# Adding an attention mask with VectorE while it reduces the row, instead of with TensorE into PSUM

## The chip, the cores and the metric

The kernel runs on one core of one Trainium2 chip. The metric is the device time of one execution in microseconds (us); for the kernel before it is the median of 3 runs.

## The reference

Three stages follow each other. The first is sliding window attention with sinks, and only this one is touched by the change: 2 batches, 8 heads, 768 positions, head size 64, everything in float32. A query sees the keys less than 128 positions behind it, and the first 4 keys.

```python
scores = scale * np.matmul(q, k.transpose(0, 1, 3, 2))
keep = is_sink | in_window
scores = np.where(keep, scores, -1000000000.0)
scores = scores - np.max(scores, axis=-1, keepdims=True)
a = np.exp(scores)
a = a / (np.sum(a, axis=-1, keepdims=True) + 1e-09)
return np.matmul(a, v).astype(np.float32)
```

The second stage turns the attention's output by the angle `x @ w_theta`, mixes tokens with two 768 x 768 matrices and adds a ReLU branch. The third is a gated block with a 512 x 1024 input matrix, a layer norm, a 768 x 768 mixing over tokens and an output matrix.

## The kernel before

Every engine has a program of its own, and semaphores order them. The attention goes over 8 blocks: four pairs of heads, and for each pair the two batches (function `pair(n, b, last, with_tok)` in the programs of TensorE, VectorE and ScalarE). A block has 6 tiles of 128 queries. Both heads of a pair lie side by side, head h on partitions 64h to 64h+63 of the transposed q and k. Tile i is scored against 128 keys (i = 0), 256 keys (i = 1) or 288 (i of 2 and more: two blocks of 128 keys, and 32 columns for the sinks).

For one tile the work passes through the engines so:

1. TensorE, `scores` (L1139): into the PSUM buffer `s_ps[i % 2]`, for each head first a matmul of the bf16 identity `ident_b` with the bf16 mask `BIAS[i]` (0 or -1e9; L1148), then three matmuls for q and k, each split in a high and a low float32r part (L1154).
2. VectorE, `maxima` (L836): per head one `tensor_reduce` with max and negation (L839) gives `neg_max`.
3. ScalarE, `exps` (L560): per head `exp(score + neg_max)` with the row's sum in its accumulator (L564).
4. TensorE, `turn_probs`: transposes of the probabilities (L1164, L1166). ScalarE copies head 0 (L581) and VectorE head 1 (L858) to SBUF, and TensorE multiplies by v (`times_v`, L1176 for the sinks, L1181).
5. VectorE, `weights` and `normalise`: the divisor (L862, L864), the product (L871).

The programs are written out by hand in an order that has the scores of tile i+2 made while tile i is transposed. In the first six blocks (`with_tok`) each of the steps i = 0 to 3 also turns a piece of the token matrices: TensorE transposes it (L1204), ScalarE writes its high part (`tok_high`, L576), VectorE its low part (`tok_low`, L853). VectorE's order in such a step is `copy_pt`, `tok_low` of the step before, `weights`, `maxima`, `normalise`; ScalarE's is `copy_pt`, `exps`, `tok_high`. TensorE's transposes of piece j wait for the low part of piece j-1.

At a block's end, q and k of the next are transposed (L1136), and ScalarE (`q_high` L551, `k_high` L558) and VectorE (`q_low` L827, `k_low` L834) split them. Scores of its tiles 0 and 1 are made between the transposes of x. These go to `x_t` by L610 (ScalarE) and L913 (VectorE), and TensorE's last transposes of k wait for both.

The first two blocks are written out on all three engines. Blocks 2 to 5 are a loop in hardware of two turns (`Fori(1, PAIRS - 1)`), in which semaphore values and addresses come from registers. Blocks 6 and 7 are written out.

GpSimd makes the identity and `ident_b` (L446), loads w_theta, and splits it with one copy (L453) and one subtraction (L455) near the start. VectorE makes the mask (L816 to L820), ahead of its first `q_low`. TensorE waits for `ident_b` before its first transpose (L1257) and for the mask ahead of its first scores (L1267).

Of the kernel before, what the change touches and what calls it, by code (L numbers as in the profile page):

```python
# [6 lines left out]
F32 = mybir.dt.float32  # L7
F32R = mybir.dt.float32r
BF16 = mybir.dt.bfloat16
I32 = mybir.dt.int32  # L10
ACT = mybir.ActivationFunctionType
ALU = mybir.AluOpType
AX = mybir.AxisListType

BATCH, HEADS, SEQ, HD = 2, 8, 768, 64
P = 128
# [8 lines left out]
PAIRS = HEADS // 2  # L25
HALFSEQ = SEQ // 2
# [3 lines left out]
SINKS = 32  # L30
WIN = 2 * P
STEP = P + SINKS
K_COLS = 2 * P + (TILES - 2) * STEP
SCALE = 1.0 / math.sqrt(HD)
NEG = 1.0e9
DEN_EPS = 1e-9
VAR_EPS = 1e-6

# [6 lines left out]
def attn_moe_gmlp(nc, q, k, v, n_sink, window, w_theta, w_tok_r, w_tok_i, w_ch, w_in, w_spatial, b_spatial,  # L45
                  w_out, out):
    ctx = ExitStack()
    with ctx:
        def sem(name):
            return ctx.enter_context(nc.semaphore(name))  # L50

        def at(name, offset, shape, dt):
            return nc.alloc_sbuf_tensor_at(name, shape, dt, offset=offset)
# [11 lines left out]
        const_at = stage_at + 2 * SEQ * 4  # L65
# [41 lines left out]
        rel = at("rel", o, [P, WIN], F32)  # L107
        col = at("col", o + 1024, [P, WIN], F32)
        keep_w = at("keep_w", o + 2048, [P, WIN], F32)
        keep_s = at("keep_s", o + 3072, [P, WIN], F32)  # L110
        keep_1 = at("keep_1", o + 4096, [P, WIN], F32)
        o += 5120
        bias_0 = at("bias_0", o, [P, P], BF16)
        bias_1 = at("bias_1", o + 256, [P, WIN], BF16)
        bias_2 = at("bias_2", o + 768, [P, SINKS + WIN], BF16)
# [8 lines left out]
        q_hi, q_lo = (at(f"q_{w}", o + 3072 * j, [P, SEQ], F32R) for j, w in enumerate(("hi", "lo")))  # L124
# [48 lines left out]
        stage = [at(f"stage{b}", stage_at + SEQ * 4 * b, [P, SEQ], F32) for b in range(2)]  # L173
        b_row = at("b_row", stage_at, [P, SEQ], F32)
        ident = at("ident", const_at, [P, P], F32)
        ident_b = at("ident_b", const_at + 512, [P, P], BF16)
        small = const_at + 768
        lims_i = at("lims_i", small, [P, 4], I32)
        words = at("words", small + 32, [P, 4], F32)
# [3 lines left out]
        neg_max = at("neg_max", small + 64, [P, 2, 2], F32)  # L183
# [11 lines left out]
        s_ps = banks[0:2]  # L195
# [4 lines left out]


        s_ident = sem("ident_made")
        s_identb = sem("ident_b_made")
        s_lims = sem("limits_loaded")
        s_iota = sem("iota_made")
        s_mask = sem("mask_steps")
        s_bias = sem("bias_made")
# [7 lines left out]
        s_qhi = sem("q_hi_ready")  # L215
# [4 lines left out]
        s_max = sem("max_ready")  # L220
# [95 lines left out]
        def ncols(i):  # L316

            return P if i == 0 else WIN + (SINKS if i >= 2 else 0)
# [21 lines left out]
        BIAS = [bias_0, bias_1] + [bias_2] * (TILES - 2)  # L340
# [91 lines left out]
        def _(pool):  # L432
            pool.memset(ident[:, :], 0.0).then_inc(s_ident, 1)
            for b in range(2):
# [7 lines left out]
                      allow_small_or_imprecise_dtypes=True).then_inc(s_iota, 1)  # L442
            pool.iota(col[:, :], pattern=[[1, WIN]], base=0, channel_multiplier=0,
                      allow_small_or_imprecise_dtypes=True).then_inc(s_iota, 1)
            pool.wait_ge(s_ident, 2)
            pool.tensor_copy(ident_b[:, :], ident[:, :]).then_inc(s_identb, 1)  # L446


            pool.wait_ge(s_k, 32)
# [95 lines left out]
        def _(act):  # L545
            def q_high(g, t, unit, src=tr_ps):

                act.wait_ge(s_tr, t + 1)
                if unit is not None:
                    act.wait_ge(s_sc, 2 * unit)  # L550
                act.activation(q_hi[:, g * HALFSEQ:(g + 1) * HALFSEQ], src[:, 0:HALFSEQ], ACT.Copy,  # L551
                               scale=SCALE).then_inc(s_qhi, 1)

            def k_high(g, t, bank=tr_ps):

# [4 lines left out]
            def exps(m, i, b):  # L560

                for h in range(2):
                    act.wait_ge(s_max, 2 * m + h + 1)
                    act.activation(probs[i % 2][:, 0:ncols(i), h], s_ps[i % 2][:, h, 0:ncols(i)], ACT.Exp,  # L564
                                   bias=neg_max[:, i % 2, h:h + 1],
                                   accum_out=sums[:, (TILES * b + i) % 4, h:h + 1]).then_inc(s_exp, 1)

            def x_high(n, j):
# [218 lines left out]
        def _(dve):  # L787
# [25 lines left out]
            dve.tensor_tensor(keep_1[:, :], keep_w[:, :], keep_s[:, :], ALU.max).then_inc(s_mask, 1)  # L813
            dve.tensor_tensor(rel[:, 0:P], keep_w[:, P:WIN], keep_s[:, 0:P], ALU.max).then_inc(s_mask, 1)
            dve.wait_ge(s_mask, 5)
            dve.tensor_scalar(bias_0[:, :], rel[:, 0:P], -1.0, NEG, ALU.add, ALU.mult).then_inc(s_bias, 1)  # L816
            dve.tensor_scalar(bias_1[:, :], keep_1[:, :], -1.0, NEG, ALU.add, ALU.mult).then_inc(s_bias, 1)
            for c, dst in ((0, 0), (P, STEP)):
                dve.tensor_scalar(bias_2[:, dst:dst + P], keep_w[:, c:c + P], -1.0, NEG, ALU.add, ALU.mult).then_inc(s_bias, 1)
            dve.tensor_scalar(bias_2[:, P:STEP], keep_s[:, 0:SINKS], -1.0, NEG, ALU.add,  # L820
                              ALU.mult).then_inc(s_bias, 1)

            def q_low(g, no, src=tr_ps):

                dve.wait_ge(s_qhi, 2 * no + g + 1)
                cols = slice(g * HALFSEQ, (g + 1) * HALFSEQ)
                dve.scalar_tensor_tensor(q_lo[:, cols], src[:, 0:HALFSEQ], SCALE, q_hi[:, cols].bitcast(F32), ALU.mult,  # L827
                                         ALU.subtract).then_inc(s_qlo, 1)

            def k_low(g, no, bank=tr_ps):  # L830
# [4 lines left out]

            def maxima(m, i):  # L836
                for h in range(2):
                    dve.wait_ge(s_sc, 2 * m + h + 1)
                    dve.tensor_reduce(neg_max[:, i % 2, h:h + 1], s_ps[i % 2][:, h, 0:ncols(i)], AX.X, ALU.max,  # L839
                                      negate=True).then_inc(s_max, 1)  # L840

            def x_low(n, j):

# [80 lines left out]
                maxima(i, i)  # L924
            for b in range(2):
                pair(0, b, False, True)
            with dve.Fori(1, PAIRS - 1) as n:
                for b in range(2):
                    pair(n, b, False, True)
            pair(PAIRS - 1, 0, False, False)  # L930
# [3 lines left out]
            with dve.If(dve.value_load(general[0:1, 0:1]) > 0):  # L934
# [11 lines left out]
                with dve.Fori(0, PAIRS) as n:  # L946
                    for b in range(2):
                        m = (2 * n + b) * TILES
                        for i in range(TILES):
# [13 lines left out]
                            for h in range(2):  # L963
# [9 lines left out]
                                                  negate=True).then_inc(s_g_max, 1)  # L973
# [54 lines left out]
            for j in range(4):  # L1028
                b, turn = j % 2, GT // 2 - 2 + j // 2
                dve.wait_ge(s_z[b], 2 * turn + 1)  # L1030
                tile = slice(GT - 4 + j, GT - 4 + j + 1)
# [94 lines left out]
        def _(pe):  # L1126
# [12 lines left out]
            def scores(m, i, pair_no):  # L1139

                pe.wait_ge(s_qlo, 2 * pair_no + i // 3 + 1)
                pe.wait_ge(s_klo, 4 * pair_no + (1, 1, 3, 4, 4, 4)[i])
                if not (isinstance(m, int) and m < 2):
                    pe.wait_ge(s_exp, 2 * m - 2)
                keys = slice(k_col(max(i - 1, 0)), k_col(max(i - 1, 0)) + ncols(i))
                tile = slice(i * P, (i + 1) * P)
                for h in range(2):
                    pe.matmul(s_ps[i % 2][:, h, 0:ncols(i)], ident_b[:, :], BIAS[i][:, :], start=True, stop=False)  # L1148

                for q_part, k_part in ((q_lo, k_hi), (q_hi, k_lo), (q_hi, k_hi)):  # L1150
                    for h in range(2):
                        rows = slice(h * HD, (h + 1) * HD)
                        last = q_part is q_hi and k_part is k_hi
                        mm = pe.matmul(s_ps[i % 2][:, h, 0:ncols(i)], q_part[rows, tile], k_part[rows, keys], start=False,  # L1154
                                       stop=last)
                        if last:
                            mm.then_inc(s_sc, 1)
# [96 lines left out]
                    turn(k_raw, 3)  # L1254

            pe.wait_ge(s_ident, 2)
            pe.wait_ge(s_identb, 1)  # L1257

            pe.wait_ge(s_q, 32)
            turn(q_raw, 0)  # L1260
# [3 lines left out]
            turn(q_raw, 3, pt_ps[:, 1, :])  # L1264
            pe.wait_ge(s_qlo, 1)
            turn(k_raw, 3)
            pe.wait_ge(s_bias, 5)  # L1267
            for i in range(2):
                scores(i, i, 0)
            pe.wait_ge(s_qlo, 2)  # L1270
# [10 lines left out]
            with pe.If(pe.value_load(general[0:1, 0:1]) > 0):  # L1281
                with pe.Fori(0, PAIRS) as n:
                    for b in range(2):
                        m = (2 * n + b) * TILES
                        pe.wait_ge(s_g_load, 96 * (2 * n + b) + 96)
                        for g in range(4):
# [4 lines left out]
                            for j in range(3):  # L1291
                                mm = pe.transpose(tr_ps[:, j * P:(j + 1) * P], (g_q_raw, g_k_raw)[g // 2][:, g % 2 * 3 + j, :],
                                                  ident[:, :])
                            mm.then_inc(s_g_tr, 1)
                        pe.wait_ge(s_g_trc, 4 * (2 * n + b) + 4)
                        for i in range(TILES):
                            for h in range(2):
                                u = 2 * (m + i) + h
                                rows = slice(h * HD, (h + 1) * HD)
# [147 lines left out]
```

## Time and profile before

| | before |
| --- | --- |
| device time, median of 3 runs (lowest to highest) | 525.67 us (524.82 to 526.9) |
| the profiled execution: span from first to last instruction | 532.6 us |
| mean granted TensorE clock in that span | 0.958 |
| busy: TensorE matmuls / weight loads | 497.1 us (93%) / 431.1 us (81%) |
| busy: VectorE / ScalarE / GpSimd | 254.8 us (48%) / 188.7 us (35%) / 123.9 us (23%) |
| chain that ended last: TensorE / VectorE / ScalarE | 76% / 11% / 5% |

The profile is one execution, another than the three timed ones. Its time outside the span isn't given, so its own time is known only as no less than 532.6 us, 5.7 us above the slowest of the timed runs. The attention takes about 197 us of the span. Busy matmuls overlap each other in the records. The chain of waits is followed back from the last instruction, and shows which work set the end in each stretch. The granted clock is the share of 2.4 GHz that TensorE was granted: 1.00 is 2.4 GHz, 0.50 is 1.2 GHz.

### The profile page before, as it was taken

To read this page: it belongs to the slowest core of one execution; us is meant where nothing else is said; L and a number is where in the kernel's file an instruction comes from. 1 tells how busy PE (TensorE), PEld (TensorE's weight loads), DVE (VectorE), ACT (ScalarE), POOL (GpSimd) and SP (SyncE) were. 2 spreads that over 40 slices of the span, in tenths; PEclk is the share of its full clock that TensorE was granted. 3 is DMA by queue.
4 is the path that set the end of the run, shared out by engine and by line. 5 is a ranking of instruction groups with operands and counts; after the bars stand their busy time and mean duration, and the time that the engine had idled before them with its cause. 6 is when DMAs were issued, how large, how long until landed. Compare 5 with 4: busy or idle time off the path is not lost.

```text
span 532.6 us, 8197 instructions
## 1 busy us (share of the span) xinstructions
PE 497.1 (93%) x2844; PEld 431.1 (81%) x2844; DVE 254.8 (48%) x591; ACT 188.7 (35%) x474; POOL 123.9 (23%) x93
## 2 busy tenths in 40 slices
PE   3899999989989997879999999999999999999997
PEld 2687877868768775659999999988888888999885
DVE  5744676767766738996000010475262540333222
ACT  2523565554644715663111111254142321110220
POOL 2500000000000002686544443000000007443442
PEclk9955999999999997897999999999999999999999
DMA  8603251651422000000420000120010110000122
GB/s 212 136 30 77 74 121 40 142 100 49 90 50 43 0 5 2 0 0 1 144 94 1 0 0 0 33 87 1 0 60 0 32 76 1 0 0 0 41 98 98
DMA packets 44527, 25.83 MB, mean 48 GB/s; under 512 B 39248, under 2 KB 39248, under 8 KB 44496
## 3 DMA queue, kind: packets, MB, share of 16 engines
q1 hardware_dynamic: 43152, 20.19, 15.1%
q0 software_dynamic: 1344, 5.24, 2.8%
q8 instruction: 17, 0.28, 0.2%
q14 instruction: 14, 0.11, 0.1%
HBM read 22.28 MB, written 3.15 MB: 48 GB/s over the span
## 4 chain that ended last, share of the span: by engine, by line
PE 76%; DVE 11%; ACT 5%; issue 5%; POOL 1%; DMA 1%; SPq 0%; DVEq 0%; ACTq 0%; POOLq 0%
PE ps L1129 18%; PE ps L1130 18%; PE ps L1131 18%; PE ps L1181 6%; PE ps L1136 4%; PE ps L1154 4%; PE ps L1164 3%; ACT probs L564 2%; PE ps L1176 2%; DVE red L1007 2%; PE ps L1148 2%; DVE neg_max L839 1%; ACT tok_hi L576 1%; DVE tok_lo L853 1%; DVE xtl L845 1%
## 5 line engine op out<-in xcount | busy, mean ns | idle before, releaser
L1129 PE MATMUL ps<-tok_hi,zl 128*128 128x384 f32 x192 | 65.4, 341 | 4.5 <-POOL zl L485 4.5
L1130 PE MATMUL ps<-tok_lo,zh 128*128 128x384 f32 x192 | 65.3, 340 | 0.0
L1131 PE MATMUL ps<-tok_hi,zh 128*128 128x384 f32 x192 | 65.2, 340 | 0.0
L564 ACT ACTIVATE probs<-ps,neg_max 128x288 f32<-128x288 f32 (+2 forms) x96 | 45.6, 488 | 38.8 <-DVE neg_max L839 38.3
L1181 PE MATMUL ps<-v_raw,p_t 128*128 128x64 f32 x352 | 52.9, 295 | 1.4 <-issue 1.4
L1181 PEld LDWEIGHTS ps<-v_raw,p_t 128*128 128x128 f32 x352 | 46.1, 203 | 8.3 <-issue 4.9
L1039 DVE TENSOR_TENSOR x_t<-ps,x_t 128x768 f32 (+1 forms) x8 | 7.7, 958 | 80.1 <-PE ps L1131 80.1
L466 POOL COPY x_sb<-xs 128x768 f32 x8 | 6.6, 827 | 163.5 <-DVE xs L871 163.5
L1129 PEld LDWEIGHTS ps<-tok_hi,zl 128*128 128x128 f32 x192 | 37.0, 193 | 4.9 <-issue 4.9
L839 DVE TENSOR_REDUCE neg_max<-ps 128x1 f32<-128x288 f32 (+2 forms) x96 | 36.0, 416 | 4.7 <-PE ps L1154 4.4
L1130 PEld LDWEIGHTS ps<-tok_lo,zh 128*128 128x128 f32 x192 | 36.9, 192 | 0.0
L1131 PEld LDWEIGHTS ps<-tok_hi,zh 128*128 128x128 f32 x192 | 36.9, 192 | 0.0
L1164 PE MATMUL ps<-ident,probs 128*128 128x128 f32 x176 | 32.4, 305 | 1.5 <-ACT p_t L581 1.3
L1129 PE MATMUL ps<-sp_hi,vl 128*128 128x384 f32 x96 | 32.2, 335 | 0.7 <-ACT gate_t L749 0.7
L1130 PE MATMUL ps<-sp_lo,vh 128*128 128x384 f32 x96 | 32.1, 334 | 0.0
L1131 PE MATMUL ps<-sp_hi,vh 128*128 128x384 f32 x96 | 32.1, 334 | 0.0
L1164 PEld LDWEIGHTS ps<-ident,probs 128*128 128x128 f32 x176 | 26.6, 209 | 3.0 <-ACT probs L564 2.2
L520 POOL TENSOR_TENSOR vl<-vn_sb,vh 128x768 fp32r<-128x768 f32 x8 | 19.5, 2444 | 38.2 <-ACT vh L717 38.2
L1107 DVE TENSOR_TENSOR mixed<-ps,b_row 128x768 f32<-128x768 f32 x8 | 7.7, 957 | 43.1 <-PE ps L1131 43.1
L858 DVE COPY p_t<-ps 128x384 f32<-128x384 f32 (+2 forms) x48 | 23.4, 488 | 9.1 <-PE ps L1166 4.8
L1129 PE MATMUL ps<-th_hi,xtl 128*128 128x512 f32 x48 | 21.2, 442 | 6.6 <-DVE red L1013 6.0
L475 POOL TENSOR_TENSOR zi_sb<-x_sb,sin_x 128x512 f32 (+1 forms) x12 | 16.4, 1368 | 29.1 <-ACT cos_x L668 29.1
(146 smaller groups left out, 1131.3 us busy)
## 6 DMA issues: line engine op xcount, KB each, us to landing
q_raw<-in_q SPq DMA_DIRECT2D x16, 192.0 KB, 3.1
k_raw<-in_k SPq DMA_DIRECT2D x16, 192.0 KB, 3.7
v_raw<-in_v SPq DMA_DIRECT2D x16, 192.0 KB, 3.2
out<-o_sb SPq DMA_DIRECT2D x12, 256.0 KB, 2.0
stage<-in_moe_w_tok_r SPq DMA_DIRECT2D x6, 384.0 KB, 3.4
stage<-in_moe_w_tok_i SPq DMA_DIRECT2D x6, 384.0 KB, 3.0
stage<-in_moe_w_spatial SPq DMA_DIRECT2D x6, 384.0 KB, 3.4
in_raw<-in_moe_w_in POOLq DMA_DIRECT2D x1, 2048.0 KB, 9.5
```

Of the source, the lines that this page charges most:

```text
L475: pool.tensor_tensor(zi_sb[:, tile, :], x_sb[:, tile, :], sin_x[b][:, :].rearrange("p (o n) -> p o n", o=1), ALU.mult).then_inc(s_z[b], 1)
L520: pool.tensor_tensor(vl[b][:, :, :], vn_sb[:, b * TILES:(b + 1) * TILES, bass.ds(n * P, P)], vh[b][:, :, :].bitcast(F32), ALU.subtract).th ...
L564: act.activation(probs[i % 2][:, 0:ncols(i), h], s_ps[i % 2][:, h, 0:ncols(i)], ACT.Exp, bias=neg_max[:, i % 2, h:h + 1], accum_out=sums[: ...
L839: dve.tensor_reduce(neg_max[:, i % 2, h:h + 1], s_ps[i % 2][:, h, 0:ncols(i)], AX.X, ALU.max, negate=True).then_inc(s_max, 1)
L858: dve.tensor_copy(p_t[i % 2][1][:, 0:pt_cols(i, 1)], pt_ps[:, 1, 0:pt_cols(i, 1)]).then_inc(s_ptc[1], 1)
L1129: pe.matmul(dst, w_lo, m_hi, start=first, stop=False)
L1130: pe.matmul(dst, w_hi, m_lo, start=False, stop=False)
L1131: return pe.matmul(dst, w_hi, m_hi, start=False, stop=last)
L1136: mm = pe.transpose(dst[:, j * P:(j + 1) * P], src[:, base + j, :], ident[:, :])
L1154: mm = pe.matmul(s_ps[i % 2][:, h, 0:ncols(i)], q_part[rows, tile], k_part[rows, keys], start=False, stop=last)
L1164: mm = pe.transpose(pt_ps[:, h, dst:dst + P], probs[i % 2][:, c:c + P, h], ident[:, :])
L1181: mm = pe.matmul(o_ps[:, cols], p_t[i % 2][h][:, c:c + P], v_raw[b][:, t, cols], start=(i < 2 and j == 0), stop=(j == len(blocks(i)) - 1 a ...
```

## The change

The mask is no longer put into PSUM by TensorE. The scores are made negated, since q is scaled by `-SCALE`, and the mask holds 0 or +1e9. VectorE adds the mask to the scores in place in PSUM and takes the row's minimum in the same instruction, which is `neg_max`. ScalarE computes `exp(-score + neg_max)`. `tensor_tensor_reduce(out, in0, in1, scale, scalar, op0, op1, accum_out)` computes `out = (in0 op0 in1) * scale` and `accum_out = reduce(out, op1)` from the starting value `scalar`.

```diff
+LARGE = 3.0e38
-            pool.wait_ge(s_ident, 2)
-            pool.tensor_copy(ident_b[:, :], ident[:, :]).then_inc(s_identb, 1)
...
                 act.activation(q_hi[:, g * HALFSEQ:(g + 1) * HALFSEQ], src[:, 0:HALFSEQ], ACT.Copy,
-                               scale=SCALE).then_inc(s_qhi, 1)
+                               scale=-SCALE).then_inc(s_qhi, 1)
...
-                                   bias=neg_max[:, i % 2, h:h + 1],
+                                   scale=-1.0, bias=neg_max[:, i % 2, h:h + 1],
...
             def maxima(m, i):
                 for h in range(2):
+                    dve.wait_ge(s_bias, 5)
                     dve.wait_ge(s_sc, 2 * m + h + 1)
-                    dve.tensor_reduce(neg_max[:, i % 2, h:h + 1], s_ps[i % 2][:, h, 0:ncols(i)], AX.X, ALU.max,
-                                      negate=True).then_inc(s_max, 1)
+                    dve.tensor_tensor_reduce(s_ps[i % 2][:, h, 0:ncols(i)], s_ps[i % 2][:, h, 0:ncols(i)], BIAS[i][:, :], 1.0,
+                                             LARGE, ALU.add, ALU.min, neg_max[:, i % 2, h:h + 1]).then_inc(s_max, 1)
...
-            with dve.Fori(1, PAIRS - 1) as n:
+            for n in range(1, PAIRS - 1):
                 for b in range(2):
                     pair(n, b, False, True)
...
-                for h in range(2):
-                    pe.matmul(s_ps[i % 2][:, h, 0:ncols(i)], ident_b[:, :], BIAS[i][:, :], start=True, stop=False)
-
                 for q_part, k_part in ((q_lo, k_hi), (q_hi, k_lo), (q_hi, k_hi)):
...
-                        mm = pe.matmul(s_ps[i % 2][:, h, 0:ncols(i)], q_part[rows, tile], k_part[rows, keys], start=False,
+                        mm = pe.matmul(s_ps[i % 2][:, h, 0:ncols(i)], q_part[rows, tile], k_part[rows, keys], start=q_part is q_lo,
                                        stop=last)
...
-            pe.wait_ge(s_identb, 1)
...
-            pe.wait_ge(s_bias, 5)
```

The scale of `q_low` and the mask's factor in L816 to L820 change sign too. VectorE's program for blocks 2 to 5 is written out; TensorE and ScalarE keep their loop.

## Rows read from the trace of the kernel before

**Rows 1.** The chain of waits up to 245 us, shares of that stretch by line.

```profile
by line: PE ps L1181 13.1%; issue 9.9%; PE ps L1136 8.7%; PE ps L1154 8.0%; PE ps L1164 6.2%; ACT probs L564 4.6%; PE ps L1176 4.2%; DVE red L1007 3.4%; PE ps L1148 3.3%; DVE neg_max L839 3.2%; ACT tok_hi L576 2.7%; DVE tok_lo L853 2.5%; DV
```

**Rows 2.** Instructions by line and shape: count, busy us, mean ns, idle before.

```profile
L839 DVE TENSOR_REDUCE neg_max<-ps 128x1 f32<-128x288 f32 x64 | 26.2, 450 | 2.9 <-PE ps L1154 2.6
...
L853 DVE TENSOR_TENSOR tok_lo<-ps,tok_hi 128x384 f32 x16 | 8.9, 558 | 8.3 <-ACT tok_hi L576 8.3
...
L1010 DVE TENSOR_TENSOR ps<-ps,red 128x512 f32<-128x512 f32 x12 | 7.7, 684 | 0.0
```

**Rows 3.** Timeline near the start: start us, us, engine, line.

```profile
16.88 4.54 POOL L455 TENSOR_TENSOR th_lo<-th_raw,th_hi 128x2048 fp32r<-128x2048 f32 x1
18.89 2.57 DVE L862 TENSOR_SCALAR den<-sums 128x2 f32<-128x2 f32 x1
```

**Rows 4.** Stretches: us, TensorE busy (count), granted clock, DMA share, GB/s.

```profile
24.00:25.00 1.00, 0.76 (x6) 0.95 0.00 0
...
52.00:53.00 1.00, 1.00 (x11) 0.89 1.34 220
```

**Rows 5.** Chain of waits, 24 to 52 us: start us, us, what.

```profile
25.64 0.48 PE ps L1148 x2
...
29.45 0.64 PE ps L1204 x3
...
46.12 0.50 ACT x_t L610
...
51.17 0.48 PE ps L1148 x2
```

**Rows 6.** Timeline of one step in block 3, in the loop.

```profile
98.41 0.82 DVE L839 TENSOR_REDUCE neg_max<-ps 128x1 f32<-128x288 f32 x2
98.90 0.52 ACT L564 ACTIVATE probs<-ps,neg_max 128x288 f32<-128x288 f32 x1 [1.16 <-DVE neg_max L839]
99.31 0.19 ACT L564 ACTIVATION_READ_ACCUMULATOR probs<-ps,neg_max 128x1 f32 x1
99.40 0.51 ACT L564 ACTIVATE probs<-ps,neg_max 128x288 f32<-128x288 f32 x1
99.88 0.49 ACT L576 ACTIVATE tok_hi<-ps 128x384 f32 x1
100.53 0.56 DVE L853 TENSOR_TENSOR tok_lo<-ps,tok_hi 128x384 f32 x1 [0.56 <-ACT tok_hi L576]
101.31 0.82 DVE L839 TENSOR_REDUCE neg_max<-ps 128x1 f32<-128x288 f32 x2
```

**Rows 7.** Timeline of part of a step in block 1, which is written out.

```profile
56.74 0.49 ACT L576 ACTIVATE tok_hi<-ps 128x384 fp32r<-128x384 f32 x1
57.32 0.55 DVE L853 TENSOR_TENSOR tok_lo<-ps,tok_hi 128x384 fp32r<-128x384 f32 x1
58.06 0.80 DVE L839 TENSOR_REDUCE neg_max<-ps 128x1 f32<-128x288 f32 x2
```

**Rows 8.** Chain of waits from block 1 to 6.

```profile
58.90 0.33 PE ps L1204 x3
...
68.54 0.50 ACT x_t L610
...
97.78 0.04 DVEq L863
...
109.24 0.11 PE ps L1148 x2
...
110.31 0.22 PE ps L1148 x2
...
113.45 0.42 PE ps L1148 x2
...
160.54 0.25 PE ps L1148 x2
```

**Rows 9.** Timeline: ScalarE's copy to x_t at the end of block 3.

```profile
111.67 0.49 ACT L610 ACTIVATE x_t<-ps 128x384 f32 x1 [0.28 <-PE ps L1136]
```

More of the change, by code:

```diff
@@ L175, in attn_moe_gmlp @@
         ident = at("ident", const_at, [P, P], F32)
-        ident_b = at("ident_b", const_at + 512, [P, P], BF16)
         small = const_at + 768
@@ L202, in attn_moe_gmlp @@
         s_ident = sem("ident_made")
-        s_identb = sem("ident_b_made")
         s_lims = sem("limits_loaded")
@@ L815, in _ @@
             dve.wait_ge(s_mask, 5)
-            dve.tensor_scalar(bias_0[:, :], rel[:, 0:P], -1.0, NEG, ALU.add, ALU.mult).then_inc(s_bias, 1)
-            dve.tensor_scalar(bias_1[:, :], keep_1[:, :], -1.0, NEG, ALU.add, ALU.mult).then_inc(s_bias, 1)
+            dve.tensor_scalar(bias_0[:, :], rel[:, 0:P], -1.0, -NEG, ALU.add, ALU.mult).then_inc(s_bias, 1)
+            dve.tensor_scalar(bias_1[:, :], keep_1[:, :], -1.0, -NEG, ALU.add, ALU.mult).then_inc(s_bias, 1)
             for c, dst in ((0, 0), (P, STEP)):
-                dve.tensor_scalar(bias_2[:, dst:dst + P], keep_w[:, c:c + P], -1.0, NEG, ALU.add, ALU.mult).then_inc(s_bias, 1)
-            dve.tensor_scalar(bias_2[:, P:STEP], keep_s[:, 0:SINKS], -1.0, NEG, ALU.add,
+                dve.tensor_scalar(bias_2[:, dst:dst + P], keep_w[:, c:c + P], -1.0, -NEG, ALU.add, ALU.mult).then_inc(s_bias, 1)
+            dve.tensor_scalar(bias_2[:, P:STEP], keep_s[:, 0:SINKS], -1.0, -NEG, ALU.add,
                               ALU.mult).then_inc(s_bias, 1)
@@ L826, in q_low @@
                 cols = slice(g * HALFSEQ, (g + 1) * HALFSEQ)
-                dve.scalar_tensor_tensor(q_lo[:, cols], src[:, 0:HALFSEQ], SCALE, q_hi[:, cols].bitcast(F32), ALU.mult,
+                dve.scalar_tensor_tensor(q_lo[:, cols], src[:, 0:HALFSEQ], -SCALE, q_hi[:, cols].bitcast(F32), ALU.mult,
                                          ALU.subtract).then_inc(s_qlo, 1)
```

## The prediction

> **What bounds the kernel now.** The page's busy shares put TensorE at 93%, but they average over stages, so I read the chain of waits for the attention alone. There the mask's matmuls (L1148) hold 3.3% of 245 us, 8.1 us, and VectorE's maxima (L839) 3.2% [rows 1]. The change takes away the first and makes the second longer, so the question is on which stretches each is on the path. The chain by stretches gives four kinds.
>
> Before 21.5 us GpSimd decides. Its subtraction for w_theta takes 4.54 us, and VectorE's small `den` instruction behind it takes 2.57 us instead of 0.16: it ends when GpSimd does [rows 3].
>
> From 24.9 to 52.1 us the granted clock is 0.50, that is 1.2 GHz [rows 4], and the chain runs through TensorE almost alone.
>
> From 70 to 157 us, in blocks 2 to 5, the steps with token pieces are a ring between VectorE and ScalarE: max of head 0, exp of head 0 (0.49 us later), exp of head 1 (0.50), `tok_hi` (0.48), `tok_lo` (0.65), the divisor and the next max (0.78). It takes 2.90 us, from 98.41 to 101.31 [rows 6]. The chain goes that way 16 times, without one L1148. Only at the blocks' ends does it go through TensorE, with 0.11 and 0.22 us of L1148 [rows 8].
>
> In block 1, and in blocks 6 and 7 without token pieces, TensorE binds, with 0.24 or 0.25 us of L1148 per tile [rows 8].
>
> **What the removal gives.** I go by the pieces of L1148 on the chain. On the ring they are worth nothing.
> - Before 21.5 us: three pieces, 1.23 us together. Worth 0, for `den` still waits for GpSimd, whose subtraction waits for a DMA and not for TensorE. The copy to `ident_b` and the two moved waits are worth 0 too: the mask stands ahead of `q_low` in VectorE's program, so TensorE's scores come after it in any case. The repeated wait for `s_bias` is always met.
> - At 1.2 GHz: five pieces, from 25.64 to 51.17 us, 2.08 us [rows 5]. There TensorE's step is over 4 us against the ring's 2.90, so all of it counts: -2.1.
> - Six transitions (into blocks 2 to 7), 0.33 us each [rows 8]. Next in line is ScalarE's `x_t` copy, which has 0.28 us of idle ahead of it [rows 9], and its `exp` comes behind the longer max (below: 0.14 us). Left are 0.28 - 0.14 = 0.14 us each: -0.8 (bounds 0 and -2.0).
> - The first scores of two blocks, about 0.4 us each [rows 8]. VectorE's `p_t` copy is next, and the max itself grows: 0.2 each, -0.4.
> - Block 1 at 2.4 GHz: two pieces, 0.49 us, against three longer maxima once the ring takes over: 0.
> - Blocks 6 and 7: six pieces like the one at 160.54 [rows 8]: -1.5. VectorE has some 2.0 us of work there in a step of 2.5, so the longer instructions fit.
>
> **What the new instruction costs.** No row shows it. It reads PSUM and the mask, writes PSUM and hands out an extreme. Two-source instructions that read PSUM take 558 ns for 384 columns and, in place, 684 ns for 512: 0.98 ns per column, so 464 ns at 288, against 450 for the reduction [rows 2]. That is 0.01 us more. The second wait costs VectorE's queue one slot, 0.04 us, as L863's does [rows 8]. Handing out the extreme costs nothing if it comes with the instruction. ScalarE's counterpart is an instruction of its own of 0.19 us, and the next starts 0.09 us after it [rows 6]. So the max becomes later by x, between 0 (reading and writing more can't be quicker) and 0.01 + 0.04 + 0.19 = 0.24 us. I take the spacing of the one counterpart there is: x = 0.01 + 0.04 + 0.09 = 0.14.
>
> The Trainium skill ("VectorE: DVE Perf Modes", section "Two Vector instructions with no wait between them") says that a Vector instruction which also writes out its accumulator is two instructions, the main one and an accumulator read. By it the lower end would drop out and the sum below would lie at 0.14 or above; if it didn't hold here, x would be 0.05. No VectorE row shows it.
>
> **What the written-out program gives.** In the loop `tok_lo` starts 0.65 us after `tok_hi`, in written-out block 1 0.58; from `tok_lo` to the max it is 0.78 against 0.74 [rows 6, 7]. So registers cost the ring 0.07 + 0.04 = 0.11 us per step, and VectorE's part of that goes in blocks 2 to 5. Sixteen passes: 16 x (0.14 - 0.11) = +0.5. This part hides most of the new instruction's price.
>
> **The sum.** -2.1 - 0.8 - 0.4 - 1.5 + 0.5 = -4.3 us. The span of 532.6 us is 6.9 above the runs' median of 525.67; I take the difference over to the median: 521.4. Ends of x: at 0 the terms are -2.1 - 2.0 - 0.8 - 0.5 - 1.5 - 1.8 = -8.7, so 517.0; at 0.24 they are -2.1 - 0.2 + 0.3 - 1.5 + 2.1 = -1.4, so 524.3. The stages behind the attention only move.
>
> **Rivals.**
>
> *The low clock lasts longer* (slower). TensorE falls to 1.2 GHz at 24.9 us, after a stretch with holes (busy 0.76 of the last microsecond), and comes back at 52.1 [rows 4], in the midst of two tiles of scores. The change takes the full-height matmuls out of just that stretch, and leaves a wider hole ahead of 21.5 us. Nothing in the rows says that it comes back at the same place. From the last token piece to `x_t` a block takes 46.12 - 29.45 = 16.67 us at 1.2 GHz and 68.54 - 58.90 = 9.64 at 2.4 [rows 5, 8]: 7.0 more, 6.7 without the masks. Its four steps add from 1 to 2 us each where TensorE takes over from the ring, or less in the lighter first ones: 10 us for one more block, 531.4. It decides once the low stretch is longer by about half a block. Against it: after 52.1 the clock stays at 1.00 through the attention.
>
> *The clock comes back earlier or isn't lost.* By the same rows block 0's end would give 6.7 and its last step some 1 more: 514.
>
> *The instruction is dearer than its parts.* Each 0.1 us on x falls on 16 ring passes, 3 of block 1 and 6 transitions: 2.5 us. The gain is gone at x = 0.31, where the 288 columns take 0.76 us with the wait. At x = 0.4 it is 527.9. For it: no such instruction is in the trace. Against: twice as long as any two-source row says.
>
> *The removed matmuls were cover only.* If the chain's 0.25 us pieces are the array's changeover to half-height weights, which stays, and the transitions are held by ScalarE, no gain is left outside the low stretch, and that one is absorbed with the clock: 525.7.
>
> **Chances.** Forecast 0.48 (517.0 to 524.3), longer low clock 0.20 (531.4), dearer instruction 0.10 (524 to 530), cover only 0.12 (525.7), better clock 0.10 (514). A measurement of this kernel tells 0.5%, 2.6 us, from no change. Below 523.0 lie 0.40 of the forecast and the better clock: faster 0.50. Within: 0.08, the cover 0.12 and 0.02 of the dear instruction: 0.22. Slower: 0.20 + 0.08 = 0.28. The range from 514 to 531 leaves out about half of the longer low clock and some of the better one.
>
> **What the new profile would show.** Right: no L1148; TensorE idle ahead of token pieces in blocks 2 to 5; ring steps of 2.9 us; blocks 6 and 7 shorter by some 0.25 us a step; from max to exp about 0.63 us; the clock's return near 50 us. Wrong: a low clock past 60 us or none at all, an instruction over 0.7 us, or steps of blocks 6 and 7 unchanged.

## The result, and the profile after

The changed kernel takes 530.87 us (median of 8 executions, 528.1 to 549.9); the kernel of before, run beside it, 525.68 us (8 executions, 524.2 to 534.7). The ratio is 1.0086 [1.006, 1.0111]: slower by 0.9%, where 521.4 us had been forecast. It is outside "no change" and just inside the upper end of the range, 531.

One thing about the executions has to be known to read what follows: those of one and the same kernel differ by how long TensorE runs at 1.2 GHz, and the ratios leave out every execution more than 1.5% above its kernel's fastest.

The profiled execution of the changed kernel took 549.85 us, its span 548.0. These are the head of its page and the lines that answer to the kernel of before's:

```profile
span 548.0 us, 8067 instructions
...
PE 511.0 (93%) x2748; PEld 442.3 (81%) x2748; DVE 260.0 (47%) x687; ACT 188.6 (34%) x474; POOL 124.5 (23%) x92
...
PEclk9856999999965558797999999999999999999999
```

The row of clocks has two deep dents: slices 2 to 4 (14 to 55 us) and slices 12 to 15 (about 151 to 206 us). The kernel of before had only the first; shallower ones (digits 7 and 8) lie behind the attention in both. In stretches of the trace (us, TensorE busy and its instructions, granted clock, DMA share, GB/s) the edges are these:

```profile
24.00:25.00 1.00, 0.51 (x4) 0.70 0.00 0
27.00:28.00 1.00, 1.00 (x8) 0.50 0.00 0
...
51.00:52.00 1.00, 1.00 (x10) 0.65 1.32 233
52.00:53.00 1.00, 1.00 (x11) 1.00 1.34 218
...
154.00:155.00 1.00, 0.78 (x4) 0.55 1.17 264
155.00:156.00 1.00, 1.00 (x8) 0.50 1.20 249
207.00:208.00 1.00, 1.00 (x3) 0.50 0.00 0
208.00:209.00 1.00, 1.00 (x4) 0.64 0.00 0
209.00:210.00 1.00, 1.00 (x6) 1.00 0.00 0
```

The first fall and the return lie half a microsecond ahead of where [rows 4] has them: 24.4 and 51.7 us. The second low stretch, from 154.1 to 208.7 us, is new. Ahead of it TensorE was busy for 0.33 of the microsecond from 151 and 0.36 of that from 153:

```profile
151.00:152.00 1.00, 0.33 (x4) 1.00 0.00 0
152.00:153.00 1.00, 1.00 (x9) 1.00 0.00 0
153.00:154.00 1.00, 0.36 (x6) 1.00 0.31 72
```

Such holes alone don't bring it: in a quick execution of the same kernel (below) TensorE is busy for 0.45, 0.88, 0.55 and 0.58 of the microseconds from 142, at the same place of the program, and the clock stays at 1.00.

What that costs stands on the chain of waits, where ScalarE's copy to `x_t` ends each block (start us, us, what):

```profile
46.02 0.50 ACT x_t L607
...
151.38 0.50 ACT x_t L607
...
181.15 0.50 ACT x_t L607
...
213.77 0.49 ACT x_t L607
```

Block 0 ends as before (46.12, [rows 5]), though three of the removed pieces, 1.12 us, lie ahead of that. They are used up by a token transpose that starts at 24.71 us and not at 24.24 (GpSimd's subtraction is 0.37 us later here), and by the fall at 24.4 and not at 24.9: the transposes from there take 1.72 us for 1.18. At 151.38 the changed kernel is 3.5 us ahead: the kernel of before has this copy at 154.93. Then blocks 6 and 7 take 29.8 and 32.6 us, where they took 19.5 and 22.6. That is +20.25 us; behind the attention 1.3 us are gained (334.2 us against 335.5). So -3.55 + 20.25 - 1.3 = +15.4, the difference of the spans (548.0 - 532.6).

The new instruction, by line and shape, and one step of block 3 in the timeline:

```profile
L837 DVE CUSTOM_DVE_ANT_0 ps<-ps,bias 128x288 f32<-128x288 f32 x64 | 28.2, 482 | 4.2 <-PE ps L1149 3.8 <-issue 0.3
L837 DVE DVE_READ_ACCUMULATOR2_ANT neg_max<- 128x1 f32 x96 | 13.6, 141 | 0.0
```

```profile
111.72 0.47 DVE L837 CUSTOM_DVE_ANT_0 ps<-ps,bias 128x288 f32<-128x288 f32 x1
...
112.10 0.14 DVE L837 DVE_READ_ACCUMULATOR2_ANT neg_max<- 128x1 f32 x1
112.10 0.50 DVE L837 CUSTOM_DVE_ANT_0 ps<-ps,bias 128x288 f32<-128x288 f32 x1
112.28 0.51 ACT L561 ACTIVATE probs<-ps,neg_max 128x288 f32<-128x288 f32 x1 [0.39 <-DVE neg_max L837]
...
113.25 0.49 ACT L573 ACTIVATE tok_hi<-ps 128x384 f32 x1
...
113.77 0.56 DVE L851 TENSOR_TENSOR tok_lo<-ps,tok_hi 128x384 fp32r<-128x384 f32 x1 [0.57 <-ACT tok_hi L573]
...
114.56 0.47 DVE L837 CUSTOM_DVE_ANT_0 ps<-ps,bias 128x288 f32<-128x288 f32 x1
```

The instruction is two: 482 ns, and a read of the accumulator of 141 ns with which the next instruction starts. From max to `exp` it is 0.56 us against 0.49 [rows 6], where 0.63 had been expected; the ring takes 2.84 us (111.72 to 114.56) against 2.90. The Trainium skill ("VectorE: DVE Perf Modes", section "Two Vector instructions with no wait between them") had said of such an instruction that it is two. By that the trace agrees; the price, 141 ns, is the trace's.

### The profile page after: what moved, and what is told of

The parts are those of the page before. It is cut to its first block, busy times and chain, and to the rows that moved or that the text cites. A ratio compares the mean times of both kernels' runs of the same rounds, so it can differ in the third digit from the quotient of the medians.

```text
span 548.0 us, 8067 instructions
## 1 busy us (share of the span) xinstructions
PE 511.0 (93%) x2748; PEld 442.3 (81%) x2748; DVE 260.0 (47%) x687; ACT 188.6 (34%) x474; POOL 124.5 (23%) x92
## 4 chain that ended last, share of the span: by engine, by line
PE 77%; DVE 12%; ACT 5%; issue 4%; POOL 1%; DMA 1%; SPq 0%; ACTq 0%; DVEq 0%; POOLq 0%
PE ps L1127 17%; PE ps L1129 17%; PE ps L1128 17%; PE ps L1176 10%; PE ps L1159 4%; PE ps L1149 3%; PE ps L1134 3%; PE ps L1171 3%; DVE red L1005 2%; ACT probs L561 2%; PE ps L1199 2%; DVE ps L1008 1%; DVE red L1001 1%; DVE red L1011 1%; DVE xtl L843 1%
## 5 line engine op out<-in xcount | busy, mean ns | idle before, releaser
L1176 PE MATMUL ps<-v_raw,p_t 128*128 128x64 f32 x352 | 62.9, 333 | 1.5 <-issue 1.5
L1176 PEld LDWEIGHTS ps<-v_raw,p_t 128*128 128x128 f32 x352 | 55.5, 239 | 9.9 <-issue 7.5
L837 DVE CUSTOM_DVE_ANT_0 ps<-ps,bias 128x288 f32<-128x288 f32 (+2 forms) x96 | 39.0, 447 | 5.3 <-PE ps L1149 4.7
L1159 PE MATMUL ps<-ident,probs 128*128 128x128 f32 x176 | 37.2, 342 | 1.8 <-ACT p_t L578 1.2
L1159 PEld LDWEIGHTS ps<-ident,probs 128*128 128x128 f32 x176 | 30.0, 217 | 3.8 <-ACT probs L561 2.4
L869 DVE TENSOR_TENSOR xs<-ps,rden 128x128 f32<-128x128 f32 x48 | 13.9, 290 | 25.5 <-PE ps L1176 25.3
```

The lines of the kernel that those rows point to most:

```text
L837: dve.tensor_tensor_reduce(s_ps[i % 2][:, h, 0:ncols(i)], s_ps[i % 2][:, h, 0:ncols(i)], BIAS[i][:, :], 1.0, LARGE, ALU.add, ALU.min, neg_ ...
L1159: mm = pe.transpose(pt_ps[:, h, dst:dst + P], probs[i % 2][:, c:c + P, h], ident[:, :])
L1176: mm = pe.matmul(o_ps[:, cols], p_t[i % 2][h][:, c:c + P], v_raw[b][:, t, cols], start=(i < 2 and j == 0), stop=(j == len(blocks(i)) - 1 a ...
```

## The experiments

Three theories stood at first. **A, the clock:** without the mask's matmuls TensorE spends more time at 1.2 GHz; at 2.4 GHz the change gains some 3 us. **B, the instruction:** the longer maximum on VectorE holds the attention, whatever the clock. **C:** VectorE's written-out program costs the time. A fourth, **H, the hole**, came up later: the clock is lost through a gap of TensorE's work near 22 us that GpSimd makes. The experiments were run in three groups, each with the kernel of before beside it: 525.75 us in the median of 28 executions (the first four experiments), 526.24 of 24 (the next four) and 526.19 of 28 (the last four).

### The kernel of before again

No edit.

> The kernel before, once more, for a look at an undisturbed execution: the page of before was taken of an execution of about 534.5 us (span 532.6), 9 us above the median. Theory A (the clock): the profile of a 525 us execution has no stretch at 1.2 GHz from 25 to 52 us, or a much shorter one, and the rest of the attention as before; span 523 to 525. Theory B (the instruction) and theory C (the written-out program) say nothing of it: the low stretch would be there in any execution, and the 9 us would lie elsewhere, spread over stages.

524.76 us in the median (10 executions, 522.84 to 536.52), ratio 0.9984 [0.9961, 1.0008]. The profiled execution took 527.05 us, and its clock is another than in the profile that the prediction read:

```profile
24.00:25.00 1.00, 0.50 (x4) 0.64 0.00 0
27.00:28.00 1.00, 1.00 (x9) 0.66 0.00 0
28.00:29.00 1.00, 1.00 (x10) 1.00 0.00 0
```

It is back at 2.4 GHz at 28 us, not at 52, as A had it. (Block 7 of this trace has another short low stretch, from 181.3 to 184.7 us, that the prediction's profile had not.) There is a difference at the start, too, that the granted clock doesn't show, but the length of the matmuls does. A group of three 128x128 transposes here (upper fence, timeline) and in the changed kernel (lower):

```profile
19.35 0.52 PE L1204 MATMUL ps<-ident,stage 128*128 128x128 f32 x3
```

```profile
19.16 0.85 PE L1199 MATMUL ps<-ident,stage 128*128 128x128 f32 x3
```

The changed kernel still runs at the pace of 1.2 GHz here, and reaches the quick one at about 21 us; in this trace of before it is reached by 18 us. That isn't the mask's matmuls alone: of the traces below that have none of them at the start, two reach it by 17.6 us (pieces, late filler), one at 27 and one after 59. Of the 88 executions of the kernel of before that ran beside the others, 61 took 528 us or less and 27 between 533 and 537, none more; with the ten here it is 68 and 30. The page that I had read was of one of the 27: a span of 532.6 us, with some 1.85 us around it 534.5.

### The changed kernel with the mask's matmuls back

```diff
+                for h in range(2):
+                    pe.matmul(s_ps[i % 2][:, h, 0:ncols(i)], ident_b[:, :], BIAS[i][:, :], start=True, stop=False)
...
-  ... k_part[rows, keys], start=q_part is q_lo,
+  ... k_part[rows, keys], start=False,
```

The copy to `ident_b` and the waits come back too. The mask is added twice here.

> The kernel after, with the mask's matmuls put back on TensorE (the mask is then added twice). TensorE has all of its old work, VectorE the new instruction and the written-out program. Theory A (the change lost by low clock that comes with the removed matmuls): 525 to 528 us, with executions spread as those of before. Theory B (the new instruction costs it): the instruction's cost comes on top of all of TensorE's old work, 531 us or more. Theory C (VectorE's written-out program costs it): 531 or more as well.

526.5 us (12 executions, 523.4 to 537.0), ratio 1.0006 [0.9982, 1.0031]. With the matmuls back the executions lie as those of before do: 8 of 12 up to 527.4, 4 from 533 to 537, none, by their times, with a second long stretch of low clock. The new instruction and the written-out program are in this kernel, so neither of them makes the loss; B would have left it. What is left of the difference is the removal.

### The kernel of before without the mask

```diff
-                for h in range(2):
-                    pe.matmul(s_ps[i % 2][:, h, 0:ncols(i)], ident_b[:, :], BIAS[i][:, :], start=True, stop=False)
...
-  ... k_part[rows, keys], start=False,
+  ... k_part[rows, keys], start=q_part is q_lo,
```

This kernel adds no mask at all; VectorE's reduction stays as it was.

> The kernel before with the mask left out altogether: no mask matmul, the plain reduction over unmasked scores, VectorE's loop as before. Only TensorE's removal is left. Theory A: no faster than before, 526 to 531 us, with executions above 535 us more often than before's and stretches at 1.2 GHz in the attention. Theory B: the gain without the price, 519 to 522 us. Theory C: 519 to 522 us as well.

530.68 us in the median of 6 executions: 519.5, 528.9, 530.6, 530.7, 532.3 and 542.1. There are too few alike for a ratio. As A had it. The removal alone does it: the one quick execution is 3.2 us below the quickest of before beside it, and the other five are 9 us or more above that quick one, where 8 of the 28 of before beside it are long; one is longer than any of before.

### The kernel of before, VectorE's program written out

```diff
-            with dve.Fori(1, PAIRS - 1) as n:
+            for n in range(1, PAIRS - 1):
```

> The kernel before, with VectorE's program for blocks 2 to 5 written out and nothing else changed. Theories A and B: 16 ring passes at up to 0.11 us less, 524 us (523.5 to 525.7). Theory C: 529 us or more, with VectorE waiting for nothing that the profile shows.

531.29 us in the median of 11: five from 520.5 to 525.1 us, six from 531.3 to 534.1. The ratio, 0.9941 [0.9916, 0.9965], rests on the five; their quickest took 520.5 us, the quickest of before beside it 522.7. The six long ones are a larger share than before's 8 of 28, and by the median alone C, 529 us or more, would stand. Against C are the five, and the kernel with the mask's matmuls back, written out too, of whose 12 executions 4 are long. Whether writing out makes the low clock more frequent these counts can't tell. The chain has the copies to `x_t` here (upper fence) and in the kernel of before again (lower):

```profile
59.41 0.50 ACT x_t L610
...
142.94 0.50 ACT x_t L610
```

```profile
59.48 0.50 ACT x_t L610
...
145.69 0.50 ACT x_t L610
```

Blocks 2 to 5 take 83.53 us against 86.21, 2.7 less; 0.11 us on each of 16 passes had been reckoned, 1.8. From `tok_hi` to `tok_lo` it is 0.51 us in this trace (86.79 to 87.30) against 0.65 in the loop [rows 6], and the ring takes 2.72 us. Against the kernel with both the new instruction and the mask's matmuls, whose blocks 2 to 5 take 85.87 us, this one shows the instruction alone: 2.34 us, or 0.146 if spread over 16 passes, where x had been 0.14. The pass itself is 2.84 us there, 0.12 more, of which 0.08 lies between max and `exp` (0.56 against 0.48) and 0.04 ahead of the max; the rest of the 2.34 falls at the blocks' starts and on one longer step.

### The changed kernel again

No edit.

> The kernel after, once more, for a look at an undisturbed execution (the page of after was taken of one of 549.85 us). Theory A (the low clock near the start is the rule once the mask's matmuls are gone): matmuls from 20 to 50 us as long as at 1.2 GHz (transposes of the probabilities near 0.42 us against 0.30), whatever clock the records state there, and full speed from about 55 us on; 528 to 531 us. Rival (the loss lies in steps at full clock): matmuls from 20 to 50 us at full speed and blocks 2 to 5 longer than the 21.1 to 21.9 us of before.

519.6, 519.7, 531.1 and 542.4 us. The profiled execution is a quick one and not of the kind that the expectation describes, with a span of 517.8 us and the granted clock at 1.00 through the attention. Its matmuls take as long as at 1.2 GHz until 27 us (a pair of the scores' matmuls takes 0.44 us at 21.68 us and 0.29 at 27.04), and then the short time. This is what the change is worth when the clock stays: 519.6 against 522.6, the quickest of before beside it, so -3.0 us. With the first 8, the changed kernel's 12 executions are 519.6 and 519.7; six from 528.1 to 531.1; and 538.8, 541.3, 542.4 and 549.9. Ten of twelve lose some 8 us or more, against 27 of 88 before. Four are beyond any of before. The second long stretch was seen in the one of 549.9 only; that the other three have one, too, is taken from their times.

### Filler matmuls in the first two blocks

```diff
+                for h in range(2 * REPS):
+                    pe.matmul(s_ps[i % 2][:, h % 2, 0:ncols(i)], ident_b[:, :], BIAS[i][:, :], start=True, stop=True)
                 for q_part, k_part in ((q_lo, k_hi), (q_hi, k_lo), (q_hi, k_hi)):
```

The scores that follow overwrite what the filler writes. Here it is one pair ahead of each of the first 12 tiles: the removed work, back in two blocks, with its result unused.

> The kernel after, with the mask's matmuls kept in blocks 0 and 1 only and as filler: the scores' first matmul overwrites what they wrote, and VectorE adds the mask as in after. Theory A: the start is back as before, with executions near 520 us (519.5 to 522) and, as with before, some near 531. Rival (the loss lies in the new instruction or in steps at full clock): 528 to 531, as after.

Missed. 534.96 us in the median of 14, ratio 1.0008 [0.998, 1.0036]. It rests on six executions, and these are 524.4 to 527.5 us rather than 520. Three lie near 535, five from 542 to 548. The profiled execution has no low clock at the start, though TensorE's hole is there (busy for 0.09 of the microsecond from 22), and a long one late:

```profile
PEclk9999999999855568977999999999999999999999
```

So the late fall doesn't need the early one, and what the first blocks are given doesn't keep it away.

### A denser filler

REPS is 3 for the first six tiles and 1 for the next two.

> As the last one, but with three times the filler in block 0 and one in the first two tiles of block 1. Theory A: 519.5 to 522 us, and fewer executions in the long form than with the single filler, since TensorE's hole at 18 to 24 us, behind GpSimd's subtraction, gets shorter. Rival: 528 to 532, the filler's own time on top.

520.22 us in the median of 12, ratio 0.9928 [0.9889, 0.9967]. Eight lie between 519.8 and 520.3, the other four at 523.2, 527.4, 530.4 and 530.7; none above. Matmuls whose result nobody reads make this kernel quicker: its median was 530.87 us over the twelve executions above, though two of the four run beside this experiment were at 519.6 too. The run doesn't tell A from H, for the filler also fills the hole: TensorE is busy for 0.97, 1.00, 1.00 and 0.80 of the microseconds from 21. Why three pairs on six tiles also keep the late stretch away, and one pair on twelve does not, no run here says.

### GpSimd's subtraction in four pieces

```diff
-            pool.tensor_tensor(th_lo[:, :, :], th_raw[:, :, :], th_hi[:, :, :].bitcast(F32),
-                               ALU.subtract).then_inc(s_th_w, 1)
+            for c in range(KC):
+                part = (slice(None), slice(c, c + 1), slice(None))
+                low = pool.tensor_tensor(th_lo[part], th_raw[part], th_hi[part].bitcast(F32), ALU.subtract)
+            low.then_inc(s_th_w, 1)
```

The rest is the changed kernel, without filler.

> The kernel after, with GpSimd's one 4.5 us subtraction for w_theta in four pieces, so that VectorE's divisor waits for a piece of about 1.1 us and not for the whole, and TensorE's hole behind it closes. If the hole keeps the clock low (theory H): most executions near 519 to 521 us. Theory A in its narrow form (it is the lacking matmuls from 11 to 18 us): the start stays slow as in after, 525 to 529 us, better by the 2 to 3 us of the hole at most.

520.13 us in the median of 8, ratio 0.9899 [0.9866, 0.9933]: five from 518.5 to 520.9, two near 530, one at 540.6. In the timeline VectorE's `den`, which GpSimd's subtraction holds, is this in the quick execution of the changed kernel (first fence) and here (second):

```profile
18.32 3.19 DVE L860 TENSOR_SCALAR den<-sums 128x2 f32<-128x2 f32 x1
```

```profile
17.21 4.97 POOL L454 TENSOR_TENSOR th_lo<-th_raw,th_hi 128x512 fp32r<-128x512 f32 x4
18.62 1.12 DVE L862 TENSOR_SCALAR den<-sums 128x2 f32<-128x2 f32 x1
```

`den` now waits for one piece (1.28 us each) and not for the whole. Elsewhere it takes 0.16 us. TensorE's gap behind it shrinks, in the changed kernel's execution of 549.85 us (first fence) and here (second):

```profile
21.00:22.00 1.00, 0.68 (x7) 1.00 0.63 138
22.00:23.00 1.00, 0.00 (x0) 1.00 0.64 255
23.00:24.00 1.00, 0.85 (x8) 1.00 0.00 0
24.00:25.00 1.00, 0.51 (x4) 0.70 0.00 0
```

```profile
21.00:22.00 1.00, 0.92 (x8) 1.00 0.77 304
22.00:23.00 1.00, 0.50 (x5) 1.00 0.11 40
23.00:24.00 1.00, 1.00 (x11) 1.00 0.00 0
24.00:25.00 1.00, 0.89 (x9) 1.00 0.03 8
```

No microsecond is empty any more, and the clock does not fall. By their times the start is lost in two of eight executions, against ten of twelve (and two of the four run beside it): for the start H fits, and A in its narrow form, 525 to 529 us, does not. But the hole alone doesn't decide: in the traces with the mask's matmuls back and with filler in two blocks TensorE is busy for 0.14 and 0.09 of the microsecond from 22, and the clock doesn't fall. The execution profiled here (span 538.8 us) has the late stretch alone, so H says nothing of that one.

The Trainium skill ("SBUF — State Buffer", section "SBUF: two separate sides") says that of a GpSimd instruction and certain VectorE instructions the one that starts first has the ports that they share for its whole length. By it pieces let `den` in sooner, and the trace agrees: 1.12 us.

### Filler in the last two blocks only

REPS is 1 for the last 10 tiles: those of blocks 6 and 7 but the first two, whose scores are made in the hardware loop.

> The kernel after, with the mask's matmuls kept as filler in blocks 6 and 7 only, where executions above 535 us lost the clock a second time. Theory A (low clock follows the removed matmuls, stretch by stretch): no execution above 535 us; two groups, near 521 (full speed from the start, 1.5 us of filler) and near 529 to 532 (slow start). Rival L (the late loss has nothing to do with the matmuls of blocks 6 and 7): a quarter or more of the executions above 537 us, as in after.

531.78 us in the median of 12, ratio 1.0002 [0.9966, 1.0039]. All are between 522.4 and 534.7; nothing as long as the late stretch occurs, which 4 of 12 had without filler, and eight still lose some 9 us, as for the early one. In its trace the holes ahead of block 6 are there (0.33 and 0.47 of the microseconds from 151 and 153) and the clock stays at 1.00. So A fits, though the quick group lies from 522.4 to 527.2 us and not near 521. It isn't shown that the filler's place matters: the denser filler near the start had no late stretch in 12 executions either.

### Both fillers and the pieces

> The kernel after with the denser filler in block 0, filler in blocks 6 and 7, and GpSimd's subtraction in four pieces. Theory A: nearly all executions at 519.5 to 521 us, none above 535. Rival L: some above 537.

521.07 us in the median of 12, ratio 0.994 [0.9915, 0.9966], all between 520.4 and 524.4, seven of them up to 521.1. By the times neither long stretch occurs; beside it, with late filler and neither the early filler nor the pieces, the early loss was in eight of 12. The filler itself costs about 2 us: the quickest is 520.4 against 518.5 with the pieces alone.

### The kernel of before, written out, with the pieces

The mask stays with TensorE's matmuls and the maximum a plain reduction. The edits are the two shown: VectorE's loop written out, and GpSimd's subtraction in four.

> The kernel before (mask by TensorE, plain reduction), with VectorE's program written out and GpSimd's subtraction in four pieces. Theory A: full-speed executions at 518.5 to 520 us (the written-out one's best 520.5 less the hole's 1 to 2), slow starts at 530 in fewer executions than the written-out kernel's 6 of 11 if the hole is what loses the clock at 25 us, in as many if it isn't; none above 535.

519.07 us in the median of 6, all between 518.6 and 521.0, ratio 0.9889 [0.9857, 0.9921], as expected: none loses the start, where six of 11 did without the pieces. The page's clock has no dent in the attention:

```profile
span 517.2 us, 8071 instructions
...
PEclk9999999999999999889999999999999999999999
```

This beats the kernel of before by 1.1% and the changed one's median, of another group of runs, by some 12 us, and has none of the change's new instruction.

### The same with filler

> The last one with two more pairs of mask matmuls, as filler, ahead of each tile's scores in block 0. Theory A: nearly all executions at 518.5 to 520.5 us, and the best median of all versions with e10's.

Missed. 522.09 us in the median of 11 (521.0 to 523.3), ratio 0.9935 [0.9916, 0.9954]. Where the mask's matmuls stand, filler only costs: 3.0 us in the median here, 2.4 between the quickest.

## Why the prediction was wrong

**The sum at full clock was near, in part by luck.** It had -4.3 us, of which -2.1 was at 1.2 GHz and so isn't there when the clock stays: -2.2. Measured between quickest executions: -3.0. By its terms (the parts come from another group of runs than the whole, from one quickest execution each, and add up to -2.5):

| Term | predicted, 2.4 GHz | measured |
|---|---|---|
| new instruction | +2.2 (16 x 0.14) | +2.34 in blocks 2 to 5; +2.9 in all (523.4 against 520.5) |
| program written out | -1.8 (16 x 0.11) | -2.7 in blocks 2 to 5; -2.2 in all (520.5 against 522.7) |
| matmuls removed | -2.7 (0.8 + 0.4 + 1.5) | -2.1 in blocks 2 to 5 (83.78 against 85.87), -1.7 in blocks 6 and 7 (40.47 against 42.14); -3.2 in all (519.5 against 522.7) |

- *The instruction:* right in size. Of its parts the accumulator read counts most, 0.08 us of a pass's 0.12. The rival of a dearer instruction falls: 482 ns, not over 700.
- *The written-out program:* mis-sized, 0.18 us a pass (2.90 to 2.72) for 0.11. The start of `tok_lo` was taken from block 1 as 0.07 us shorter than in the loop; it became 0.14 shorter.
- *The removal:* mis-sized where it was weighed against ScalarE. From the last `tok_hi` of a block to the `x_t` copy it is 8.76 us with the matmuls and the new instruction, and 8.44 in the changed kernel: 0.32 us at each transition, nearly all of the 0.33 on the chain, and not 0.28 - 0.14 = 0.14. The new instruction takes nothing from it (8.77 with the plain reduction). From the `x_t` copy to the next block's first `tok_hi`, where the first scores lie, the four blocks are 0.8 us shorter together (15.58 against 16.38), and not 0.4. "Cover only" falls with this.
- *Blocks 2 to 7 together:* 128.53 us in the profile of before (86.39 and 42.14, all at 1.00), 124.25 in the changed kernel's quick execution, so -4.3 where these terms give -2.2. That the whole is only -3.0 means that more than 1 us is lost elsewhere; no quick execution of the kernel of before was profiled to say where.
- *The ring:* 2.84 us where 2.93 followed, mostly by the same 0.07 a pass.

**The step that failed is the clock's.** The sum put it as "At 1.2 GHz: five pieces, from 25.64 to 51.17 us ... so all of it counts: -2.1", with the low stretch at its place and length, and then "I take the difference over to the median". Both halves were wrong. The pieces themselves were rightly sized, as the account of block 0 above shows for the first three. But the profile read was of an execution of the kind that 27 in 88 are, with the long low stretch, so its -2.1 us isn't in the median of before at all. And in the changed kernel the loss is no longer the exception but the rule, 10 executions in 12, 8 us or more each. The rival "the low clock lasts longer", given 0.20, named the mechanism and its place, that the full-height matmuls go from just that stretch, and gave 531.4; measured were 530.9. But its form was another: in the profiled execution the stretch isn't longer than in the profile of before (27.3 us in both), it comes more often. The sign set for it, "a low clock past 60 us", came true by the second stretch; two signs of the forecast, ring steps of 2.9 us (2.84) and a return near 50 us (51.7), came true beside it. And the argument against it, that the clock stays at 1.00 behind 52 us, held for that one profile: two other traces with the mask's matmuls have 3.4 and 6.8 us of low clock in block 7, and in the changed kernel's profiled execution, and by their times in three more of the 12, blocks 6 and 7 run at 1.2 GHz, a loss that no text of mine had.

**What stays open.** Which feature of TensorE's work decides whether the clock falls or returns is not settled. What is shown: the removal of the mask's matmuls brings the loss, and with them back it is as frequent as before; three pairs of matmuls of no use in block 0, or a shorter gap from 21 to 25 us, go with most of the early losses gone. That late filler takes away the late loss fits, but isn't shown, for early filler did so too. The early loss has at least two forms, a late rise and a fall behind the gap, and their shares weren't counted, as each kernel left one trace or two. A hole of the same size comes with a fall in some traces and without one in others. Not explained are the one pair on twelve tiles with its five late losses, and the three executions of eight that lose in spite of the pieces. The changed kernel with VectorE's loop kept wasn't tried, nor the kernel of before with the pieces and its loop.

## What to carry to other kernels

Before taking differences from a profile, set its execution's own time beside the median of the runs: here it was 9 us off, and with it went a whole stretch at half clock. Matmuls that look cheap may be what keeps TensorE at 2.4 GHz between half-height products and transposes, so after removing some, look at all executions and at the row of clocks, not at the median alone. Try to close the gap ahead of such a loss: cutting one GpSimd instruction in four, with a loop written out, gave more than the change that was meant to.

## What the runs showed of the hardware

**A granted clock of 1.00 isn't always 2.4 GHz.** The kernel of before without the mask has no low clock on record from 20 to 50 us, and yet its matmuls there take as long as at 1.2 GHz. One stretch of it, and a group of instructions between 25 and 45 us:

```profile
30.00:40.00 10.00, 10.00 (x42) 1.00 0.14 42
```

```profile
L1161 PE MATMUL ps<-ident,probs 128*128 128x128 f32 x12 | 3.2, 421 | 0.0
```

Only after 59 us do its matmuls take the short time. The same group in the changed kernel's quick execution, between 30 and 45 us:

```profile
L1159 PE MATMUL ps<-ident,probs 128*128 128x128 f32 x14 | 2.4, 288 | 0.0
```

421 ns against 288, at the same 1.00. Its first `x_t` copy comes at 46.21 us, as in the executions with a recorded low clock, and at 38 us in that quick one. All profiles read 1.00 up to the first recorded fall, though their first matmuls are of the long kind. So a matmul of known shape is the surer clock. Two of the changed kernel's six middle executions (528.1 and 528.7 us) have a mean clock of 0.99 too, and so have four of the eight long ones with late filler (531.6 to 532.8 us); I take them for this form, but none of them was profiled.

**The low stretches of the attention came in few lengths.** The early one is 27.3 us long in all three traces that have it long (24.9 to 52.2 us before, 24.4 to 51.7 after, 24.2 to 51.5 with late filler), and 3.4 us in two (24.3 to 27.7 us, the kernel of before again and written out). The late one is 54.6 us long in all three traces that have it (after, filler in two blocks, pieces), and begins each time 2.7 to 3.1 us behind the start of block 5's `x_t` copy. Two traces have a short one in block 7, 3.4 us (the kernel of before again) and 6.8 us (written out).

**A loop on VectorE cost more than I had read.** 0.18 us of a step of 2.90, most of it at the start of one two-source instruction (0.65 us behind `tok_hi` in the loop, 0.51 written out).
